# Three PSUM banks instead of two for relu's results, and a swapped opening order for the third stream of the last down projection

## What is computed

```python
xn = x / rms * rms_g
x  = (silu(xn @ w_gate) * (xn @ w_val)) @ w_out          # d_ff 1536

h = x @ w_in                                              # d_ff 2048
relu6 = np.clip(h + 3.0, 0.0, 6.0)
g = h * relu6 / 6.0
return g @ w_out
```

## Time and profile before

| | |
|---|---|
| median of 3 runs | 1710.63 us (1709.11 to 1716.69) |
| profiled execution | 1708.24 us |
| its span, first to last instruction | 1706.4 us |
| outside the span | 1.84 us |
| granted TensorE clock, mean | 0.99 of full speed |
| PE busy | 1658.9 us, 97% |
| DVE busy | 1041.6 us, 61% |
| ACT busy | 868.7 us, 51% |
| POOL busy | 738.1 us, 43% |

### The profile page before, as it was taken

How to read it: one execution, slowest core, us unless ns; L and a number is a source line. 1 busy time by engine, 2 the same in 40 slices (tenths; PEclk the granted TensorE clock), 3 DMA queues, 4 the chain that set the end, 5 groups by cost and what they waited for, 6 DMA issues and landing times.

```text
span 1706.4 us, 31468 instructions
## 1 busy us (share of the span) xinstructions
PE 1658.9 (97%) x12263; PEld 1606.0 (94%) x12264; DVE 1041.6 (61%) x1405; ACT 868.7 (51%) x1375; POOL 738.1 (43%) x706
## 2 busy tenths in 40 slices
PE   8898999999999999999999999999999999999999
PEld 5788888999999999999999999999999999999999
DVE  4776778767755555664555776656666764444443
ACT  4655666664544444454444665555545644433442
POOL 5642434438786666432120476676566510010010
PEclk9898999999999999999999999999999999999999
DMA  9575666635476555888998856556557976666664
GB/s 177 128 186 134 158 161 174 167 104 176 153 238 209 199 195 178 306 282 307 323 326 286 302 215 231 198 185 230 212 188 260 372 258 200 205 221 202 204 222 130
DMA packets 323556, 366.98 MB, mean 215 GB/s; under 512 B 178960, under 2 KB 288272, under 8 KB 320208
## 3 DMA queue, kind: packets, MB, share of 16 engines
q1 hardware_dynamic: 310400, 329.97, 60.5%
q0 software_dynamic: 8544, 33.56, 5.9%
q10 hardware_dynamic: 4464, 1.44, 0.5%
HBM read 200.80 MB, written 164.10 MB: 214 GB/s over the span
## 4 chain that ended last, share of the span: by engine, by line
PE 79%; DVE 4%; issue 4%; ACT 2%; DMA 2%; DVEq 0%; ACTq 0%
PE bx L906 12%; PE by L906 12%; PE bx L908 11%; PE by L908 11%; PE bx L907 11%; PE by L907 11%; PE att L908 2%; PE att L907 2%; PE att L906 2%; DVE tx L1409 1%; PE att L874 1%; PE att L832 1%; DVE ub L1431 1%; DMA hl_d<-u_scratch 1%; DMA hl_b<-h_scratch 1%
## 5 line engine op out<-in xcount | busy, mean ns | idle before, releaser
L906 PE MATMUL by<-tx,wr 128*128 128x384 f32 x840 | 290.3, 346 | 8.3 <-DVE ub L1431 7.3
L906 PE MATMUL bx<-tx,wr 128*128 128x384 f32 x840 | 289.1, 344 | 5.2 <-ACT gb L1091 2.9
L908 PE MATMUL bx<-tx,wr 128*128 128x384 f32 x840 | 282.1, 336 | 0.0
L908 PE MATMUL by<-tx,wr 128*128 128x384 f32 x840 | 282.0, 336 | 0.0
L907 PE MATMUL bx<-tx,wr 128*128 128x384 f32 x840 | 282.0, 336 | 0.0
L907 PE MATMUL by<-tx,wr 128*128 128x384 f32 x840 | 281.9, 336 | 0.0
L1457 DVE TENSOR_TENSOR hl_d<-hl_d 128x1536 fp32r<-128x1536 f32 x84 | 147.6, 1790 | 119.0 <-ACT hl_d L1171 118.9
L1457 DVE TENSOR_TENSOR hl_b<-hl_b 128x1152 fp32r<-128x1152 f32 x84 | 116.5, 1399 | 111.2 <-ACT hl_b L1171 110.4
L906 PEld LDWEIGHTS by<-tx,wr 128*128 128x128 f32 x840 | 158.5, 189 | 18.5 <-DVE ub L1431 12.9
L1171 ACT ACTIVATE hl_d<-hl_d 128x1536 fp32r<-128x1536 f32 x84 | 122.4, 1482 | 99.2 <-DMA hl_d<-u_scratch 99.2
L906 PEld LDWEIGHTS bx<-tx,wr 128*128 128x128 f32 x840 | 158.5, 189 | 12.2 <-issue 5.8
(11 more groups left out here) (183 smaller groups left out, 4415.5 us busy)
## 6 DMA issues: line engine op xcount, KB each, us to landing
hl_d<-u_scratch SPq DMA_DIRECT2D x84, 768.0 KB, 4.3
hl_b<-h_scratch SPq DMA_DIRECT2D x84, 576.0 KB, 5.8
u_scratch<-ut SPq DMA_DIRECT2D x48, 576.0 KB, 3.7
h_scratch<-ht SPq DMA_DIRECT2D x36, 576.0 KB, 3.6
u_scratch<-ub SPq DMA_DIRECT2D x96, 192.0 KB, 3.0
u_scratch<-ub SPq DMA_DIRECT2D x48, 384.0 KB, 2.5
h_scratch<-vb SPq DMA_DIRECT2D x72, 192.0 KB, 3.4
h_scratch<-vb SPq DMA_DIRECT2D x36, 384.0 KB, 3.1
```

Of the source, the lines that this page charges most:

```text
L906: pe.matmul(dst, w_hi, m_hi, start=start, stop=False, skip_group_check=not opens)
L908: return pe.matmul(dst, w_lo, m_hi, start=False, stop=stop, skip_group_check=not opens)
```

## The change

relu 2 to 7 go round three banks, `att[0]`, `att[1]`, `att[2]`, by (i - 2) % 3. The result that has to be read before relu i writes is now that of relu i - 3 instead of i - 2 (for i = 2, 3, 4, the one of relu 5, 6, 7 of the step before), and `used` is changed to match. Bank `att[2]` used to be the one that stream 2 opens first in the last down projection. That stream now has its two banks the other way about, so o = 0 opens `att[3]` and o = 1 opens `att[2]`, and PE gets one new wait, in step 66, o = 1, stream 2, for the last relu's reader.

```diff
@@ bank(m, st, role)
         i = (m + {"a": 0, "c": 1, "b": 1}[role]) % 2
         if m < D0:
             return (bx, by)[st][:, i, 0:N]
-        return (bx, by, att[:, AB:AB + 2])[st][:, i, 0:256]
+        return (bx[:, i], by[:, i], att[:, AB + 1 - i])[st][:, 0:256]
@@ relu_to(i)
-        return rt[:, :] if i < 2 else att[:, i % 2, 0:N]
+        return rt[:, :] if i < 2 else att[:, (i - 2) % 3, 0:N]
@@ accumulator_free(m, o, st)
             if o == 1 and opened:
                 pe.wait_ge(*c21_free(m - 1, st))
+            if o == 1 and m == D0 and st == 2:
+                pe.wait_ge(u_done, u_no(D0 - 1, U22, 1))
@@ relu(m, i)
-            used = 8 * c + (-6, 1, -1, 0, 3, 4, 5, 6)[i]
+            used = 8 * c + (-6, 1, -2, -1, 0, 3, 4, 5)[i]
```

## The result

The changed kernel takes 1699.30 us (median of 7 runs, 1692.59 to 1702.52), the kernel before 1710.63 (7 runs, 1708.69 to 1716.69). The ratio is 0.993, 95% interval 0.9913 to 0.9948, so it is about 12 us faster by the ratio, and 11.3 by the medians. The forecast was 1707.5, with a range of 1702 to 1712. The direction was right, the size was not: the gain is more than three and a half times the 3.1 us that were summed up.

A forecast was written before the change was run, and what follows sets the result against it. The prediction took DVE, held up by POOL, to bound the fill steps. Relu 7's earlier start was to win 0.63 us a round, 3.1 us over five rounds, all else 0: 1710.63 to 1707.5 us, range 1702 to 1712.

The forecast's parts named there:

- What bounds the kernel: Second up projection: DVE bounds the fill steps, delayed by its own work, ACT's high parts and POOL; 2.7 us a round.
- That is all there is to win here: Around the fill steps of rounds 0 to 4: 2.7 us lost a round, 13.5 us in all.
- Only relu 7 of the fill steps counts: Relu 7 loses its wait there and starts at 1144.11, not 1144.52; relu 2 to 6 and other waits give 0.
- Fill 1 gets ahead of POOL by 0.05 us: In a fill step, fill 1's low part starts at 1145.49, ahead of POOL's sum at 1145.54, and takes 0.96 us.
- The next starts at 1147.26, 0.04 ahead of fill 2. POOL goes first: At fill 2 POOL's next sum beats DVE's low part, which takes 1.8 us; 0.63 us gained a round, 3.1 in all.
- The chances: Whole kernel: forecast 0.60, POOL first or no effect 0.23, DVE ahead in both 0.11, slower 0.06.
- the other side of the tie: Rival: DVE also wins at fill 2, which takes 0.96; most or all of 13.5 us won, 1697; chance 0.11.
- Swap: Third stream of the last down projection: the same matmuls and readers on the other of two banks cost 0.
- The new wait: PE's wait in step 66, o = 1, third stream: taken as 0, at most 0.2 us; last relu6_times ends 0.78 earlier.
- Slower, with DVE passed by two sums: Rival, fill steps: two POOL sums pass a waiting low part, 0.97 us more each; put at 1713, up to 1722; chance 0.06.

The follow-up runs named there:

- the kernel with DVE 0.01 us later: The changed kernel with a one-column memset on DVE ahead of the low part of fill 2 in each fill step; 1705.61 us, ratio 0.9987.

## Why the prediction was wrong

*What bounds the kernel: right for the fill steps.* The 2.7 us a round around them, 13.5 us in all, were there to win: with every tie won by DVE a round takes 58.2 to 58.3 us. "That is all there is to win here" was not right. The stage had 16.8 us of stops, and about 2.2 of them stand in steps 63 and 64, behind the end of the window of the earlier trace rows; holding POOL back there wins them (363.95). And PE does wait in the steps right behind the fill steps: the third wait of each round, at 1155.56 in the earlier trace rows, is in slot 1 of such a step. That cost the sum nothing, since with relu 7 held and all other relus free nothing is gained (366.21).

*Only relu 7 of the fill steps counts: right.* It alone gives the gain, and without it there is none.

*Fill 1 gets ahead of POOL by 0.05 us: right.* It is 0.04 ahead in rounds 1 to 4, takes 0.96, and POOL's sum takes 1.80.

*"The next starts at 1147.26, 0.04 ahead of fill 2. POOL goes first": this step failed.* It failed by the size of the lead. The displaced POOL sum ended 0.88 us after the low part (1087.80 + 1.80 against 1087.76 + 0.96), and not 0.86 as read from the one at 1148.89. The earlier trace rows already had the 0.88 (518.85 + 1.82 against 518.83 + 0.96), in the case that was like this one, with DVE just ahead. The next POOL sum was then 0.00 to 0.02 ahead in rounds 1 to 4 and not 0.04, and DVE got through; in round 0 it was 0.01 ahead and POOL went first, and that round gained what was forecast. Once DVE had got through, fills 3 and 4 met POOL in the same way and won as well, so that the low parts took 0.95 and not 1.8, and the round gained 2.7 us and not 0.6. The sum itself was sound for the case that it assumed: the kernel with DVE 0.01 us later measures 3.1 us, the term of the prediction.

*The chances: the larger mistake.* A lead of 0.04 us, put together from several rows that are given to 0.01 us, was called the likeliest case at 0.60, and the other side of the tie, worth another 10 us, got 0.11. The prediction had the mechanism, the place and the price of that case, "most or all of the 2.7 a round", and left it out of the range. Before the change the same tie stood at 0.04 for POOL (1150.60; the prediction has 0.05), which was the argument against it; but that one repeats itself in each round, while the new one was an extrapolation. An error of 0.02 to 0.04 us was enough to turn it. An even chance for either side, and a range down to 1695, is what rows of that resolution could carry. Why four rounds went DVE's way and one POOL's, at much the same recorded lead, stays open.

*Swap: 0, right. The new wait: nearly 0, right.* Its cover of 0.78 us was that of one run. In the kernel with the swap alone PE is held for 0.2 us, the bound that was given. In the changed kernel the last `relu6_times` ends at 1339.08 + 1.01 = 1340.09 and the third stream starts at 1340.16. The next matmul starts 0.21 us later in place of 0.12, so PE is held for 0.1 us:

```profile
1339.08 1.01 DVE L1480 SCALAR_TENSOR_TENSOR ub<-att,ub 128x384 f32<-128x384 f32 x2
```

```profile
1340.16 0.37 PE L908 MATMUL att<-wr,hl_d 128*128 128x256 f32 x1
1340.37 0.28 PE L909 MATMUL att<-wr,hl_d 128*128 128x256 f32 x1
```

*Slower, with DVE passed by two sums: not seen* in any fill step of the changed kernel or of the ten experiments. It stays in step 64, where DVE's weight split still takes 4.71 us in the changed kernel. Why two sums pass it there, and none of the low parts in the fill steps, was not found; holding them back removes it.

## What to carry to other kernels

Where two engines exclude each other for whole instructions, look at who starts first and by how much; a wait that has nothing to do with either may set it, and the price is that of all the instructions that follow, not of the wait. If the lead in the forecast is put together from several rows and comes out at a few times their last digit, treat both outcomes as even and give both their full price. Then take the chance out of it, on the engine with spare time (POOL here). Semaphore waits hold the order whatever the starts, and left 0.3 us a round here (58.6 against 58.24); one tiny instruction left nothing, but only moves the start, by 0.05 us.

## What the runs showed of the hardware

- DVE with two SBUF inputs and a POOL sum took turns in every fill step: the later one's recorded time is its own plus what it waited. A POOL sum that had to wait (1.02 us alone) ends 0.86 to 0.88 us after the low part, and a low part that had to wait (0.96 alone) ends 0.96 us after POOL's recorded end less 0.15. The Trainium skill (SBUF — State Buffer, "SBUF: two separate sides") says that the two lock one pair of ports for a whole instruction and that the first to start gets it. These rows agree down to about 0.02 us and not below. In the fill steps of the nine kernels in which no wait holds POOL there, take the low parts that started within 0.06 us of a POOL sum: POOL went first whenever its recorded start was more than 0.023 us ahead, and DVE whenever its own was ahead. In between both happened: DVE won with a start 0.01 us *behind* (1089.56 against 1089.55) and lost with one 0.01 us behind (1029.27 against 1029.26).
- A memset of one column ahead of it, 0.06 us in the record, moved the next DVE instruction by only 0.01 us; the kernel with it took 7.3 us more in the stage.
- Front to back the same kernel varies more than this stage: the part ahead of step 42 took 970.6 to 977.4 us in twelve profiled runs in which nothing there had been changed. The granted clock of that part was 0.99 in the shortest and 0.97 in the longest, and 1.00 in the stage in both.
